# A gated feed-forward stage that takes its rows in the order of the experts

## The reference

```python
attn_out = _attn_ref(q, k, v, i_gate, f_gate, o_gate)      # recurrent attention, 8 heads of 40
x = attn_out.transpose(0, 2, 1, 3).reshape(3072, 320)

# one expert of 8 for each token, F = 1024
logits = x @ w_gate
e_idx = argmax(logits, axis=1)
probs = exp(logits - logits.max(-1)); probs /= probs.sum(-1) + 1e-09
gate_w = probs[arange(N), e_idx]
eom = 1 / (1 + exp(-(x @ w_output_gate)))
for e in range(8):
    mask = e_idx == e
    h = maximum(x[mask] @ w1[e], 0)
    out[mask] = gate_w[mask, None] * eom[mask, e, None] * (h @ w2[e])

# a dense gated block, F = 1536
rms = sqrt(mean(x * x, axis=-1) + 1e-06)
xn = x / rms * rms_g
g = xn @ w_gate
result = (g * sigmoid(g) * (xn @ w_val)) @ w_out
```

## Time and profile before

| | |
|---|---|
| time, median of 3 runs | 909.55 us (909.12 to 910.09) |
| the profiled execution's own time | 914.29 us |
| its span, first to last instruction | 912.5 us |
| granted TensorE clock, mean over the span | 0.964 |
| TensorE busy with matmuls | 849.8 us (93%) |
| VectorE, ScalarE, GpSimd busy | 509.3, 394.0, 110.7 us |
| chain that ended last: TensorE | 85% |
| moved by DMA | 109.37 MB, mean 120 GB/s |

### The profile page before, as it was taken

How to read it: one execution, slowest core, us unless ns; L and a number is a source line. 1 busy time by engine, 2 the same in 40 slices (tenths; PEclk the granted TensorE clock), 3 DMA queues, 4 the chain that set the end, 5 groups by cost and what they waited for, 6 DMA issues and landing times.

```text
span 912.5 us, 18039 instructions
## 1 busy us (share of the span) xinstructions
PE 849.8 (93%) x6301; PEld 743.1 (81%) x6301; DVE 509.3 (56%) x1060; ACT 394.0 (43%) x714; POOL 110.7 (12%) x151
## 2 busy tenths in 40 slices
PE   5999999915999999999994999999999999999997
PEld 2777777615999999999993788888888888888886
DVE  4466566555788787878772344354354354453432
ACT  4444444404777767677761232232232233233122
POOL 4234454340000000000001100100100100100000
PEclk8899999966999999999997999999999999999999
DMA  6354445258889999999961100100100100100000
GB/s 166 89 146 129 147 140 165 72 200 279 251 266 262 266 269 279 264 253 291 296 203 37 30 1 1 58 1 1 58 0 0 58 0 0 58 0 2 28 1 29
DMA packets 76567, 109.37 MB, mean 120 GB/s; under 512 B 11380, under 2 KB 55284, under 8 KB 76516
## 3 DMA queue, kind: packets, MB, share of 16 engines
q1 hardware_dynamic: 72036, 98.20, 36.7%
q0 software_dynamic: 2304, 7.88, 2.6%
q10 hardware_dynamic: 2176, 2.62, 0.9%
HBM read 92.21 MB, written 16.47 MB: 119 GB/s over the span
## 4 chain that ended last, share of the span: by engine, by line
PE 85%; issue 5%; DMA 3%; ACT 2%; POOL 2%; DVE 1%; ACTq 1%; SPq 1%; POOLq 0%; DVEq 0%
PE psum L1419 42%; PE psum L1494 5%; PE psum L1495 5%; PE psum L1496 5%; PE psum L1443 4%; PE psum L1445 4%; PE psum L1444 4%; PE psum L1279 3%; PE psum L1330 2%; PE psum L1353 2%; PE psum L1306 2%; PE psum L1298 2%; PE psum L1299 1%; DMA w_raw<-w 1%; PE psum L1411 1%
## 5 line engine op out<-in xcount | busy, mean ns | idle before, releaser
L1242 DVE TENSOR_TENSOR gated_lo<-gated,gated_hi 128x512 fp32r<-128x512 f32 x72 | 49.9, 693 | 185.7 <-ACT gated_hi L807 185.7
L802 ACT ACTIVATE sigm_sb<-psum 128x512 f32<-128x512 f32 x72 | 43.0, 598 | 255.8 <-PE psum L1419 255.8
L1419 PE MATMUL psum<-nT_hi,w_gv_hi 128*128 128x512 f32 x432 | 125.1, 398 | 2.6 <-DVE nT_lo L1229 2.6
L1419 PE MATMUL psum<-nT_lo,w_gv_hi 128*128 128x512 f32 x432 | 124.5, 396 | 0.0
L1419 PEld LDWEIGHTS psum<-nT_lo,w_gv_hi 128*128 128x128 f32 x432 | 81.5, 189 | 19.9
L1419 PEld LDWEIGHTS psum<-nT_hi,w_gv_hi 128*128 128x128 f32 x432 | 79.0, 189 | 16.9 <-DVE nT_lo L1229 2.8
L1419 PE MATMUL psum<-nT_hi,w_gv_lo 128*128 128x512 f32 x288 | 90.6, 396 | 0.0
L635 POOL DMA_INDIRECT c_rows<-y_by_slot,slot_idx x24 | 22.8, 948 | 555.8 <-DMA y_by_slot<-y_tile 286.3
L1494 PE MATMUL psum<-w_out_hi,gated_hi 128*128 128x320 f32 x288 | 89.8, 312 | 0.0
L1495 PE MATMUL psum<-w_out_lo,gated_hi 128*128 128x320 f32 x288 | 89.1, 309 | 0.0
L1496 PE MATMUL psum<-w_out_hi,gated_lo 128*128 128x320 f32 x288 | 89.0, 309 | 0.0
(11 more groups left out here) (222 smaller groups left out, 1571.5 us busy)
## 6 DMA issues: line engine op xcount, KB each, us to landing
w_raw<-w SPq DMA_DIRECT2D x38, 640.0 KB, 6.9
w_raw<-w SPq DMA_DIRECT2D x38, 512.0 KB, 4.5
w_raw<-w SPq DMA_DIRECT2D x76, 128.0 KB, 5.1
kv_tok<-tok SPq DMA_DIRECT2D x24, 324.0 KB, 4.4
qk_sb<-qk SPq DMA_DIRECT2D x48, 160.0 KB
y_by_slot<-y_tile SPq DMA_DIRECT2D x12, 321.0 KB, 7.3
og_tok<-o_tok SPq DMA_DIRECT2D x24, 160.0 KB, 2.2
x_tile<-x_by_expert SPq DMA_DIRECT2D x12, 320.0 KB, 2.9
```

The lines of the kernel that those rows point to most:

```text
L802: nc.scalar.activation(sigm_sb[f % 2][:], bank[2 * (f % 2)][:], ACT.Sigmoid).then_inc(sig_ready, 1)
L1242: dve.tensor_tensor(gated_lo[f % 4][:], gated[f % 2][:], gated_hi[f % 4][:].bitcast(F32), ALU.subtract).then_inc(hv_lo, 1)
L1419: m = mm(dst, w, x, start=(n == 0), stop=(n == len(terms) - 1))
```

## The change

- Each row that is scattered to `x_by_expert` carries two more numbers, the gate factor and the token's number: `y_tok` is one tensor with rows of 322 numbers. They are made for each group of four blocks inside the attention stage, by VectorE (`gate_begin`, `gate_end`) and ScalarE (`gate_exp`). The computation between steps 0 to 3 of the experts is gone.
- The tiles' results are stored densely, in the order of the experts, to `y_sorted`; VectorE works out the first row of each tile's store after the other tables (`store_table`, `stori`). A later store writes over the unused rows of an earlier one, so each store waits for the one before.
- Before each store SyncE loads the two carried numbers of the tile's rows from `x_by_expert` to the end of `y_tile`'s rows, and waits for them.
- The last stage reads tiles of 512 sorted rows with plain DMAs on SyncE's queue (`c_load`). The first is issued ahead of the loads of tile 17; its variance, root and normalisation stand ahead of the last steps of the experts, and its turn inside the last tile's second product, after three quarters of it. The warm-up matmuls are gone.
- The results are scattered to `out` by GpSimd, four indirect DMAs for each tile (`tokens`).
- `c_rows` is normalised in place; one VectorE operation of 384 columns replaces two of 320 and 64.

```diff
@@ SyncE
             def expert_store(j, w):
+                row = sp.value_load(rowi[0:1, bass.ds(j, 1)], min_val=0, max_val=IDLE)
+                to = sp.value_load(stori[0:1, bass.ds(j, 1)], min_val=0, max_val=NTOK)
+                xr = x_by_expert[bass.ds(row, w), :].rearrange("(s p) n -> p s n", p=P)
+                yr = y_sorted[bass.ds(to, w), :].rearrange("(s p) n -> p s n", p=P)
+                wait(sp, e_stored, 16 * j)
+                sp.sem_inc(sync_turn, 1)
+                sp.dma_start(y_tile[:, 0:w // P, DM + 1:YW], xr[:, :, DM:XW]).then_inc(meta_in, 16)
                 sp.wait_ge(e_copied, 2 * j + 2)
                 sp.wait_ge(e_squared, 2 * j + 2)
                 sp.sem_inc(sync_turn, 1)
-                row = j * TE if w == TE else NFULL * TE - NFULL * TS + j * TS
-                sp.dma_start(y_by_slot[bass.ds(row, w), :].rearrange("(s p) n -> p s n", p=P), y_tile[:, 0:w // P]).then_inc(e_stored, 16)
+                sp.wait_ge(meta_in, 16 * j + 16)
+                sp.sem_inc(sync_turn, 1)
+                sp.dma_start(yr, y_tile[:, 0:w // P]).then_inc(e_stored, 16)
+
+            def c_load(t):
+                yr = y_sorted[bass.ds(t * TC, TC), :].rearrange("(s p) n -> p s n", p=P)
+                sp.dma_start(c_rows[:, :, 0:DM], yr[:, :, 0:DM]).then_inc(c_in, 16)
+                sp.dma_start(c_rows[:, :, DM:CW], yr[:, :, DM - TAIL:YW]).then_inc(c_in, 16)
...
-            with sp.Fori(NFULL + 2, NTE) as j:
+            with sp.Fori(NFULL + 2, NTE - 2) as j:
+                expert_loads(j, TS)
+                expert_store(j - 2, TS)
+            sp.wait_ge(e_stored, 16 * FIRST_STORES)
+            c_load(0)
+            for j in range(NTE - 2, NTE):
                 expert_loads(j, TS)
                 expert_store(j - 2, TS)
             expert_store(NTE - 2, TS)
             expert_store(NTE - 1, TS)
-
-            with sp.Fori(0, NTC) as t:
-                sp.wait_ge(o_copied, SUB * t + SUB)
-                sp.dma_start(out.rearrange("(b c p) n -> c p b n", b=B, c=NC)[bass.ds(t, 1)].rearrange("c p b n -> (c p) b n"), out_rows[:]).then_inc(o_stored, 16)
-            sp.wait_ge(o_stored, 16 * NTC)
+            sp.wait_ge(e_stored, 16 * NTE)
+            with sp.Fori(1, NTC) as t:
+                sp.wait_ge(c_idx, t)
+                sp.wait_ge(ct_made, t)
+                sp.sem_inc(sync_turn, 1)
+                c_load(t)
@@ GpSimd
+            def tokens(t):
                 for s in range(SUB):
+                    pool.wait_ge(o_copied, SUB * t + s + 1)
+                    pool.wait_ge(c_idx, t + 1)
+                    pool.sem_inc(pool_turn, 1)
                     pool.indirect_dma_start(
+                        out=out[:, :], out_offset=bass.IndirectOffsetOnAxis(ap=slot_idx[:, s:s + 1], axis=0),
+                        in_=out_rows[:, s, :], in_offset=None).then_inc(o_stored, 16)
@@ ScalarE
+            def gate_exp(g):
+                act.wait_ge(below_made, g + 1)
+                nc.scalar.activation(exp_below[:], below_top[:], ACT.Exp).then_inc(below_exp, 1)
+                act.wait_ge(own_made, g + 1)
+                nc.scalar.activation(gate_sum[:, 1], gate_sum[:, 0], ACT.Exp, scale=-1.0).then_inc(own_exp, 1)
...
+            with act.Fori(NFULL + 1, NTE - 2) as j:
+                e_step(j, TS, TS)
             root(0)
+            e_step(NTE - 2, TS, TS)
+            for r in range(4):
+                h_high(NTE - 1, r, TS)
             c_high(0)
+            e_out(NTE - 1, TS)
@@ VectorE
+            def gate_begin(g):
+                group = slice(B * g, B * g + B)
+                dve.tensor_tensor(gate_own[:], all_logits[:, group, E:2 * E], all_onehot[:, group], ALU.mult).then_inc(route_step, 1)
+                rt[0] += 1
+                dve.tensor_tensor(below_top[:], all_logits[:, group, 0:E], top_logit[:].unsqueeze(2).to_broadcast([P, B, E]),
+                                  ALU.subtract).then_inc(below_made, 1)
+                dve.wait_ge(route_step, rt[0])
+                dve.tensor_reduce(gate_sum[:, 0], gate_own[:], AX.X, ALU.add).then_inc(own_made, 1)
+
+            def gate_end(g):
+                slots = slice(B * g % NY, B * g % NY + B)
+                dve.wait_ge(below_exp, g + 1)
+                routed(dve.tensor_reduce(gate_sum[:, 2], exp_below[:], AX.X, ALU.add))
+                routed(dve.tensor_scalar(gate_sum[:, 3], gate_sum[:, 2], 1e-9, None, ALU.add))
+                dve.wait_ge(own_exp, g + 1)
+                routed(dve.scalar_tensor_tensor(out=gate_sum[:, 4], in0=gate_sum[:, 1], scalar=1.0, in1=gate_sum[:, 3],
+                                                op0=ALU.add, op1=ALU.mult))
+                if g * B >= NY:
+                    for n in range(B * g - NY, B * g - NY + B):
+                        dve.wait_ge(scattered[n], 16)
+                dve.reciprocal(y_tok[:, slots, DM], gate_sum[:, 4]).then_inc(scale_ready, 1)
+                dve.tensor_copy(y_tok[:, slots, DM + 1], token_id[:, B * g:B * g + B]).then_inc(ids_made, 1)
...
+            with dve.Fori(NFULL + 1, NTE - 2) as j:
+                e_step(j, TS, TS)
             c_variance(0)
+            e_step(NTE - 2, TS, TS)
+            dve.wait_ge(gain_in, 32)
             c_normalise(0)
+            for r in range(4):
+                h_low(NTE - 1, r, TS)
             c_low(0)
@@ TensorE
-            def expert_out(j, w):
+            def expert_out(j, w, then=None):
                 wait(pe, e_squared, 2 * j)
                 for f in range(NF1):
                     r, a = f // 2, f % 2
+                    if f == 6 and then is not None:
+                        pe.wait_ge(h_lo, 4 * j + 3)
+                        then(0)
...
+            hidden(NTE - 1, TS)
+            expert_out(NTE - 1, TS, c_turn)
             pe.wait_ge(h_lo, 4 * NTE)
-            pe.wait_ge(c_in, 16 * SUB)
-            keep_warm(12)
-            c_turn(0)
             tile(0, False)
```

## The result

The changed kernel takes **969.32 us** (median of 4 runs, 967.28 to 971.38) against 909.82 for the kernel before (4 runs, 909.12 to 911.25): ratio 1.0652, 95% interval 1.0625 to 1.0679. Slower, as forecast, and inside the range; 16 us above the number. The profiled execution has a span of 965.5 us against 912.5, so +53.0. A ratio is taken over the fast runs of both kernels alone, while the medians printed are those of all runs, so a ratio is not always the quotient of two medians.

What follows compares the result with a forecast made beforehand. The experts' stage was taken to stand on TensorE and DMA limits together. SyncE's queue +59.3, passage −16.5, clock −1.5 and end +2.1 sum to +43.4, giving 953 us; its own range 937 to 977, 8-in-10 range 924 to 975.

Steps and rivals of the forecast that it cites:

- The decisive step: SyncE's queue, experts' stage: the small load lands 0.3 us after w2, holding up the store and all loads behind it.
- The term of SyncE's queue: Experts' stage: SyncE's wait for the small load before each store makes x load 18 late by 59.3 us, head's 1.0 included.
- The full cycles: Experts' stage, x load to x load for a full tile: twelve cycles of 18.4 us against 15.4.
- upper bound, "+15.0": Small load landing 15.0 us after the x load: cycles of 19.9 and 17.6 us, +83 us, 977 us in all.
- The half cycles: Experts' stage, tiles of 128 rows: four cycles of 16.1 us against 11.0, plus 2.5 for the early load of 512 rows.
- The passage: From the last expert tile's second product to the last stage's first matmul: 7.5 us instead of 24.05, −16.5.
- The clock's −1.5: Start of the last stage: without the long hole the clock stays up and the first six or so matmuls aren't slow, −1.5 us.
- tiles still 67.3 apart: Last stage: plain loads replace gathers, transposes and matmuls stay, so tile spacing stays 67.3 us, cost 0.
- The end: Very end of the kernel: four GpSimd scatters replace one store, last landing at 914.6 against the span's 912.5, +2.1 us.
- Attention and head: Attention stage: small steps per group covered by VectorE's waits, cost 0; only the sixth group delays the first x load, +1.0 us.
- The rival "covered altogether": Experts' stage: loads run far enough ahead, so only head, passage and end count; −14.9, 895 us; chance 0.07.
- The rival "overtakes": First rival: small load passes queued w2, back in 2.5 us, about +10.7; 904 us; chance 0.12.

Runs made afterwards that it cites:

- before_waits_for_w2: The kernel before, with SyncE waiting ahead of each store until the w2 halves already issued have landed, no DMA added: 985.80 us, ratio 1.0794.
- before_small_load: The kernel before, with a 2 KB load into an unread buffer issued and awaited ahead of each store: 985.15 us, ratio 1.0790.
- own_slots: The changed kernel, with each tile's carried numbers loaded right behind its x rows into their own slot and stored by a separate small DMA: 900.68 us, ratio 0.9855.
- small_ahead_of_w2: The changed kernel, with its small load issued between the w1 and w2 loads instead of behind w2: 915.36 us, ratio 1.0052.
- before_turned_first: The kernel before, with nT_hi and nT_lo allocated ahead of c_rows and c_normed in SBUF: 908.66 us, ratio 0.9957.
- own_slots_late_passage: own_slots with the last stage's first load, normalisation and turn put back where the kernel before has them, warm-up included: 913.48 us, ratio 1.0033.
- late_passage_again: own_slots_late_passage run once more, on one chip with own_slots_again: 912.75 us, ratio 0.9997 to the kernel before.
- own_slots_again: own_slots run once more on another chip, beside late_passage_again and plain_end_again: 899.82 us, ratio 0.9866 to the kernel before.
- plain_end_again: Second run of own_slots with the last tile's 512 rows stored as one plain block by SyncE instead of four scatters: 894.94 us, ratio 0.9810 to the kernel before.

## Why the prediction was right, and where its sizes were off

**The decisive step held.** "The small load lands with w2, and everything behind SyncE's wait is late by that": the landing at X+14.2, the stalls in before_waits_for_w2 and before_small_load, and own_slots, in which the stall is gone and 69 us with it, show it from three sides. small_ahead_of_w2 adds a fourth: with w1 ahead of it, the load lands with w1.

**The term of SyncE's queue was mis-sized: +59.3 forecast, +71.5 measured,** both for x load 18. The full cycles are what was off. I took w2's landing at X+13.2 on the ground that a queue that has stood still is emptier ahead of it, though the two rows before me said +13.9 and +14.7. Over the twelve full cycles of the changed kernel the second w2 half lands at +14.6 in the mean, and in the kernel before, where SyncE waits for no load, at +14.7. Standing still bought nearly nothing. With the small load at +14.7 and 5.0 behind it (forecast: +13.5 and 4.9) the cycle is 19.7; this is the whole excess over the 18.4. ScalarE's wait for the late store's landing, which the prediction didn't see, has no part in it that shows: beside its waits for the small load (92.3 us from 225 to 530) SyncE has three others there, 7.6 us in all, and each of them ends before the small load is even issued. Between the rows and a reason to go below them, the rows were right: the prediction's upper bound, "+15.0", was nearer than its number.

**The half cycles came out (+23.2 for +23.3) by luck.** Two errors cancel. The small load lands at +14.1 in them, not at +13.5, which makes the first two cycles 17.05 and 16.84 us and not 16.1. And the early load, for which I had added 2.5, costs some 0.5: from the small load's landing to the next x load it is 3.1 us in its cycle and 2.6 in the two before.

**The passage** was right (−17.2 for −16.5), and so was what carries it: the turn inside the product, the copy under the last quarter.

**The clock's −1.5** came out against this trace of the kernel before: tile 0 takes 66.4 us from its first matmul to its output copies against 69.0, of which 1.0 is the shorter matmuls. But it is not a fixed price of the hole. With holes of 20 to 26 us, two traces show it (69.0 in the kernel before and 68.1 in before_turned_first, where a later tile takes 67.4 and 66.7), and five don't: own_slots_late_passage and late_passage_again have 66.5 like the changed kernel, the three kernels with a wait added have 67.5 for 67.4. In own_slots_late_passage the granted clock is back up at 495.4, ahead of the first matmul. The clock also falls in the stalls of the experts' stage (0.79 over the half tiles); that it costs nothing there, since SyncE paces them, was argued and not tested.

**The last stage: "tiles still 67.3 apart" was wrong.** They are 66.33 apart, 5.1 us over the five tiles behind the first. Some 70% of it comes from the place of four buffers, which I hadn't thought to be part of the change; the rest is open.

**The end was too small:** +2.1 forecast, +6.8 measured in the spans; 4.9 by the times of own_slots_again and plain_end_again. Issue and landing together came near: 5.1 us from the copies' start to the last scatter's issue and 2.5 to its landing, 7.6 for the 7.2 forecast (the term's own numbers give 914.5, not 914.6). What it missed is that the span doesn't end at the last landing: 4.4 us of GpSimd's DRAIN and the end of the program follow.

**Attention and head:** the eight small steps a group cost nothing that shows; x load 2 comes 2.7 us earlier, not 1.0 later. This is a difference between executions: in the five traces of the kernel before and of what was built on it, this load is issued between 228.3 and 232.8, in the nine traces of the changed kernel and of what was built on it between 225.7 and 232.2. A cost of 1.0 can't be told from that.

**The rival "covered altogether"** (895 us) is, in effect, own_slots at 900: the same terms with the end's size put right (+4.7 more) and the last stage's −6 against 6 us lost around the half tiles (x load 18 at 459.90 for 457.76, and 4.0 us more from there to the second product). **The rival "overtakes"** is refuted for a load behind w2 on the same queue. small_ahead_of_w2, where the load lands at X+10.9 in the mean of the sixteen cycles and the time is 0.5% above the kernel before, is near the point of balance that the prediction put at X+10.8. The rival let 3 us of slack take up part of the delay; there is none: x load 18 comes 17.1 us late there, and the last second product 17.0. The first rival also stood for the 2 us of a lone DMA. The trace has them only where nothing else is in flight: 1.6 and 1.7 us for the last two tiles' loads. The Trainium skill ("DMA: Bandwidth & Descriptors", section "Anatomy of one DMA — SWDGE (gpsimd) path"), which the prediction quoted for them, gives its figure for the path of GpSimd's DMAs, and this load is SyncE's.

## What to carry to other kernels

A wait of the issuing engine for its own fresh DMA costs not that DMA's bytes but all bytes issued ahead of it, and then delays all that is issued behind it. Count the queue's content at the point of issue, and issue small loads that are needed soon ahead of the bulk, a tile early, into slots of their own. A second queue gave no earlier landing here; it only freed SyncE from issuing the load, so that it could go out earlier. When a landing is to be estimated, take it from the rows. When an engine idles in several places of a chain, read the waits of the DMA-issuing queue before those of the compute engines.

## What the runs showed of the hardware

- A load of 2 KB lands 2.6 to 3.8 us after its issue behind 0.4 MB of x rows (own_slots), 4.2 to 6.0 behind w1 (small_ahead_of_w2), 4.6 to 7.3 behind w2 (the changed kernel; 6.4 to 8.7 in before_small_load), and 4.6 to 8.5 from a queue of its own. 1 KB with nothing else in flight takes 1.6 and 1.7.
- After four GpSimd scatters at the end 4.4 us pass from the last landing to the span's end, 4.0 of them GpSimd's DRAIN (own_slots); after a plain store 0.8.
- The same matmul of 512 columns takes 389, 392 or 396 ns in the median by where buffers lie in SBUF, at a granted clock of 1.00 (changed kernel, before_turned_first, kernel before; the step from 392 to 389 isn't isolated).
